# Attention and a gated MoE layer on one core: the portions in which the values' matmuls are queued

## What is computed

```python
scores = scale * np.matmul(q, k.transpose(0, 1, 3, 2))
psi_rel = np.log1p(np.abs(rel))
psi_i = np.log1p(np.maximum(pos[:, None].astype(np.float32), 1.0))
x = (psi_rel / psi_i)[..., None]
h = np.maximum(x @ w1 + b1, 0.0)
bias = h @ w2
scores = scores + bias.transpose(2, 0, 1)[None, :, :, :]
scores = scores - np.max(scores, axis=-1, keepdims=True)
attn = np.exp(scores)
attn = attn / (np.sum(attn, axis=-1, keepdims=True) + 1e-09)
return np.matmul(attn, v).astype(np.float32)
...
gate = 1.0 / (1.0 + np.exp(-(x @ w_gate)))
val = x @ w_val
return (gate * val @ w_out).astype(np.float32)
```

## Time and profile before

| | before |
|---|---|
| median of 3 runs | 822.9 us (821.3 to 824.1) |
| the profiled execution | 825.04 us |
| its span, first to last instruction | 823.2 us |
| TensorE busy | 782.6 us (95%) |
| VectorE busy | 332.0 us (40%) |
| ScalarE busy | 338.0 us (41%) |
| GpSimd busy | 194.9 us (24%) |
| values' matmuls (L882), share of the chain that ended last | 10% |
| mean granted clock of TensorE | 0.987 |

### The profile page before, as it was taken

One profiled execution on the slowest core, in us unless ns is written; L12 is line 12 of the kernel. 1 busy time (PEld: TensorE's weight loads), 2 busy tenths in 40 slices (PEclk: granted clock), 3 DMA queues, 4 the chain that ended last, 5 costly groups with the idle time before them and its releaser, 6 DMA issues.

```text
span 823.2 us, 13263 instructions
## 1 busy us (share of the span) xinstructions
PE 782.6 (95%) x5008; PEld 627.8 (76%) x5008; DVE 332.0 (40%) x797; ACT 338.0 (41%) x683; POOL 194.9 (24%) x362
## 2 busy tenths in 40 slices
PE   5684999999999999999989999999999999999998
PEld 2232666666666666669978998999899889989996
DVE  5894766666666666633320221123022202211220
ACT  5794666666666666643321221122022212212210
POOL 0000666646545545668400000000000000000000
PEclk9998999999999999999989999999999999999999
DMA  6684233242242233213322000100010010000001
GB/s 157 167 204 129 57 102 84 72 106 62 67 121 60 66 85 84 62 55 98 115 76 77 1 1 14 64 1 1 27 52 1 14 64 1 1 26 14 1 2 38
DMA packets 89152, 49.91 MB, mean 61 GB/s; under 512 B 60928, under 2 KB 80512, under 8 KB 89088
## 3 DMA queue, kind: packets, MB, share of 16 engines
q1 hardware_dynamic: 89088, 49.06, 21.9%
HBM read 28.98 MB, written 9.44 MB: 47 GB/s over the span
## 4 chain that ended last, share of the span: by engine, by line
PE 84%; DMA 5%; DVE 3%; ACT 3%; POOL 2%; SPq 1%; issue 1%; POOLq 0%; DVEq 0%; ACTq 0%
PE f_ps L950 18%; PE g_ps L900 15%; PE u_ps L900 15%; PE v_ps L882 10%; PE so_ps L816 9%; PE ty_ps L829 4%; PE tx_ps L841 3%; PE so_ps L811 2%; DVE feats L656 2%; DMA w_raw<-in_w_gate 2%; DMA x_raw<-in_w_out 2%; PE so_ps L764 2%; POOL w L480 1%; DMA bias<-bias_rows 1%; ACT feats L524 1%
## 5 line engine op out<-in xcount | busy, mean ns | idle before, releaser
L559 ACT ACTIVATE probs<-neg_scores,neg_max 128x576 f32<-128x576 f32 x144 | 110.6, 770 | 93.0 <-DVE neg_max L671 93.0
L900 PE MATMUL g_ps<-x_h,w 128*128 128x384 f32 x576 | 146.6, 335 | 1.2 <-DVE hid L733 1.2
L900 PE MATMUL u_ps<-x_h,w 128*128 128x384 f32 x576 | 146.3, 334 | 0.0
L733 DVE TENSOR_TENSOR hid<-u_ps,sig 128x384 f32<-128x384 f32 x72 | 40.1, 557 | 244.7 <-PE u_ps L900 244.7
L671 DVE CUSTOM_DVE_ANT_0 neg_scores<-so_ps,bias 128x576 f32<-128x576 f32 x144 | 104.0, 756 | 75.8 <-PE so_ps L816 54.6
L463 POOL TENSOR_SCALAR probs<-probs,recip 128x512 f32<-128x512 f32 x128 | 89.0, 695 | 187.6 <-DVE recip L685 187.6
L900 PEld LDWEIGHTS g_ps<-x_h,w 128*128 128x128 f32 x576 | 103.9, 188 | 2.3 <-DVE hid L733 1.6
L900 PEld LDWEIGHTS u_ps<-x_h,w 128*128 128x128 f32 x576 | 103.9, 188 | 0.5 <-issue 0.5
L620 ACT ACTIVATE h_h<-hid 128x384 fp32r<-128x384 f32 x72 | 37.9, 527 | 149.0 <-DVE hid L733 149.0
L900 PE MATMUL g_ps<-x_l,w 128*128 128x384 f32 x288 | 96.3, 334 | 0.0
L900 PE MATMUL u_ps<-x_l,w 128*128 128x384 f32 x288 | 96.2, 334 | 0.0
(11 more groups left out here) (68 smaller groups left out, 989.3 us busy)
## 6 DMA issues: line engine op xcount, KB each, us to landing
bias<-bias_rows SPq DMA_DIRECT2D x64, 144.0 KB
x_raw<-attn_transposed SPq DMA_DIRECT2D x6, 768.0 KB, 4.6
out<-out_sb SPq DMA_DIRECT2D x18, 256.0 KB, 2.0
q_raw<-in_q SPq DMA_DIRECT2D x32, 128.0 KB, 2.6
k_raw<-in_k SPq DMA_DIRECT2D x32, 128.0 KB, 2.5
v_main<-in_v SPq DMA_DIRECT2D x32, 128.0 KB, 2.3
w_raw<-in_w_gate SPq DMA_DIRECT2D x12, 256.0 KB, 2.9
w_raw<-in_w_val SPq DMA_DIRECT2D x12, 256.0 KB, 2.9
```

The source lines that it names most:

```text
L559: nc.scalar.activation(probs[s % RING][:, place, :], neg_scores[s % 2][:, place, :], ACT.Exp, bias=neg_max[:, stat(s, place)], scale=-1.0, ...
L733: nc.vector.tensor_tensor(hid[f % 2][:, :], u_ps[f % 3][:, 0:CH], sig[f % 2][:, :], ALU.mult).then_inc(gated, 1)
L900: last = nc.tensor.matmul(bank[f % 3][:, 0:CH], w[:, f, part, i, t, :], x[:, t, :], start=m == 0, stop=m == len(terms) - 1)
```

## The change

The same tiles are multiplied in other portions. Group 0: tiles 0 to 2 at m=4 and tiles 3 and 4 at m=0 of the next pair, where it was 0 and 1 at m=4, 2 and 3 at m=0, and 4 at m=1. Group 1: all five tiles at m=2 of the next pair, where it was 0 to 2 at m=2 and 3 and 4 at m=3. The call ahead of the transposes of m=1 goes.

```diff
-        VALUE_SLOTS = {4: (0, 0, (0, 1)), 0: (1, 0, (2, 3)), 1: (1, 0, (4,)), 2: (1, 1, (0, 1, 2)), 3: (1, 1, (3, 4))}
+        VALUE_SLOTS = {4: (0, 0, (0, 1, 2)), 0: (1, 0, (3, 4)), 2: (1, 1, (0, 1, 2, 3, 4))}
...
             for s in range(STEPS + DRAIN):
                 pair, m = divmod(s, SPP)
-                back, group, tiles = VALUE_SLOTS[m]
-                of, c = pair - back, s - LAG
+                back, group, tiles = VALUE_SLOTS.get(m, (0, 0, ()))
+                of, c = pair - back if tiles else -1, s - LAG
                 if s < STEPS:
                     scores(s)
-                if m == 1 and of >= 0:
-                    values(of, group, tiles)
...
-                if m != 1 and of >= 0:
+                if of >= 0:
                     values(of, group, tiles)
```

## The result

The changed kernel takes 827.87 us in the median of 6 runs (826.54 to 830.18), the kernel before, with it on the same chip, 822.46 (821.3 to 824.1). The ratio is 1.0071, with a 95% interval of 1.0056 to 1.0086: slower by 5.4 us, where 5.2 was forecast. The profiled execution took 830.2 us (span 828.4).

The account below looks back on a forecast made before the run. TensorE, busy throughout steady attention, was taken as the bound. Fourteen pairs at +0.34 us (+4.8), first pair +0.43, last +0.92 and the end -0.9 gave +5.2 us: 828.1 from the 822.9 median, range 825.4 to 831.4.

Parts of the forecast that it names:

- m=1: Attention step of each steady pair losing its portion of one tile: -0.58 us, to 2.85, just above the 2.79 floor.
- the tails' copy: ScalarE copy that the transposes of m=1 wait for: ready at 1.14 against 1.17 us, priced at nothing, bounds 0 to +0.15 a pair.
- m=2: Attention step of each steady pair getting two more tiles of 320 columns in one portion: +1.06 us, to 5.13.
- m=3: Attention step losing two tiles and a portion: -0.74 us instead of -1.23, since the next scores wait for shifts until 2.79.
- m=4: Attention step getting one tile of 256 columns, +0.43, and waiting for ScalarE's move, +0.17: together +0.60 us, to 3.77.
- ScalarE's move: Move of m=1, which frees the bank for the transposes of m=4: late there, +0.17 us a pair, bounds 0 and +0.17.
- the rival with gains: "Only the portions count": decides if m=3's second shift ends before 2.30 us after the scores' start; 817.5 us, 5%.
- The last pair: Last attention pair, its m=1 already at the floor: taking the tile out saves nothing, so this pair costs +0.92 us.
- the end: After the attention loop: values done ahead of the gate part, weight load 0.9 us earlier, bounds -0.6 and -2.3.
- Only the portions count: Rival, whole attention: m=3's shifts done before TensorE returns, two portion starts saved a pair, 5.1 us plus 0.3; 817.5 us; 5%.
- Gain and loss balance: Rival: the move of m=1 doesn't delay m=4 (-2.4) and attention's end returns 2.3 us (-1.4): 824.3 us, no measurable change; 12%.
- More is late: Rival: m=1's transposes miss the tails' copy, with an echo in m=2, +4.2 us: 832.3; or a chunk meets transfers worse; 10%.

Follow-up runs that it names:

- earlier move: Against the changed kernel, ScalarE's move of m=1 stands between the two exponentials of m=3 instead of behind them; 825.27 us, 1.0043 to the kernel before.
- group 0's part: Against the kernel before, only the first 256 queries' values regrouped: tiles 0 to 2 at m=4, 3 and 4 at m=0; 818.9 us, ratio 0.9963.
- group 1's part: Against the kernel before, only the other 320 queries' values regrouped into one portion at m=2; 828.63 us, ratio 1.0083.
- group 0 at once: Against the kernel before, the first 256 queries' five tiles in one portion at m=0, the other 320 queries unchanged; 818.83 us, ratio 0.9959.
- three: Changed kernel with row step's scores in other banks, ScalarE's move between m=3's exponentials, values copy ahead of them; 819.39 us, 0.9967 to the kernel before.

## Why the prediction was right

**The bound.** TensorE had no idle microsecond in the steady pairs, so every term was to be paid in full, and was.

**m=1** was to give 0.58: it gave 0.58, without a wait. The margin of 0.03 before the tails' copy held: the copy ends at 208.00 (207.68+0.32), 0.99 us after the scores' start at 207.01, and the transposes started at 208.19, 1.18 after it. The upper bound of 0.15 was not needed.

**m=2** was to cost 1.06 and cost 1.08: five tiles of 320 took 2.84 us. Over 14 pairs this makes the 0.3 us by which the forecast was short.

**m=3** was to give back 0.74 instead of 1.23, by the row of the first pair: 2.79 was forecast and measured. A bare step in the trace of the kernel before was the whole evidence. The 2.30 for TensorE's own account was a little high: with the shift's wait lifted the step took 2.21. No term of the sum hangs on it.

**m=4** was to cost 0.60: 3.77 was forecast and measured. The 0.17 of ScalarE's move went away alone in the kernel with the earlier move.

**The tie of the two waits was not seen.** The prediction has the shift's wait (0.49 of m=3) and the move's 0.17 as two prices that add up. As a sum this is right. As a cause it is half right: with the shift's wait lifted nothing is gained, since ScalarE's move ends 4.30 us after the start of m=3 in any case, and the transposes that need it start at 4.44. What m=3 gives back then, m=4 takes: 0.58 us either way. The prediction's sentence that only the shift's end decides the rival with gains (before 2.30) was therefore too little: the move, VectorE's move and the copy of the values behind them would have had to be early too. With a bare m=3, the shift's wait and ScalarE's move both lifted, the pair was 17.76, no shorter than before the change.

**The last pair and the ends.** The last pair's m=1 stayed at 2.79, as forecast. For the end, the last scores, the last store and the load of piece 14 in the changed kernel (it answers to the earlier trace rows):

```profile
362.26 1.24 PE L811 MATMUL so_ps<-qk 128*128 128x288 f32 x4 [0.41 <-DVE neg_max L671]
...
376.65 0.34 SPq L366 DMA_DIRECT2D attn_transposed<-x_half  x1
377.03 0.43 SPq L350 DMA_DIRECT2D w_raw<-in_w_gate  x1
```

The load came 14.77 us after the last scores instead of 15.20, although m=4 has become 0.60 longer in between: 1.03 us earlier, where 0.9 was forecast. The prediction's sign for it (0.9 us earlier against the last scores) was worded wrongly: against them it is 0.43, since the 0.60 of m=4, which the sum counts by itself, lies behind them. Of the 1.03, 0.2 was lost again in the loads and splits on the way to the outputs (49.56 us from that load to the outputs, 49.36 before).

**The rivals.** "Only the portions count" came to pass in group 0's part, where TensorE never waits in the steady pairs; there two portions instead of three gave 0.16 us a pair. The Trainium skill (TensorEngine Tiling (Array Packing), Key Properties) states that changing the tiling mode drains TensorE. The trace agrees in direction: a portion less saved 0.16 us a pair. That the drain is what a start costs, no run here shows. In group 1's part one portion less has the same gain on TensorE's own account, and the waits behind it cost four times that (0.51+0.16 = 0.67 us a pair). "Gain and loss balance" had the end of attention give 2.3; it gave 1.0. "More is late" did not occur.

## What to carry to other kernels

When an engine is the bound and its queue mixes two kinds of work, the second kind may be cover for a round trip through the other engines; before taking it out of a step, look for a step that already runs bare, at the start or the end of the loop, and read its length. A saving of 0.16 us per portion is worth taking where the step stays longer than its round trip (here 2.79 us with two shifts; with one shift a step of 2.19 us had no listed wait). And before lifting a wait, ask which one is ready next: here four stood one behind the other (the shift, VectorE's move, ScalarE's move, ScalarE's copy), and the first one lifted alone was worth nothing.

## What the runs showed of the hardware

Executions of one kernel lie up to 4.6 us apart (the kernel before, 820.28 to 824.83 in one series), and the faster ones tend to have the higher mean granted clock (0.992 against 0.988). In the profiles three places differ that no experiment touches. The first is the start of attention: the first pair's scores of m=1 come between 78.63 and 80.71 us, and why is left open here. The other two go with the granted clock, both behind a stretch in which TensorE idles. One is m=2 of the first pair, behind a wait of 7.7 to 9.3 us that falls in the bias table's transfers: with the same queue it took from 2.78 to 3.63 us in these profiles. The other is the first chunk's outputs, behind a wait of 2.4 to 3.0 us for the output weights. They are 108 instructions in every kernel; the chain of waits gives them, before and in group 0's part,

```profile
420.32 27.53 PE f_ps L950 x108
```

```profile
416.20 24.74 PE f_ps L948 x108
```

and the same 108 take 24.52 us in later chunks. In the kernel before the granted clock was 0.50 from 422 to 426 us:

```profile
422.00:426.00 4.00, 4.00 (x10) 3.03 (x10) 0.52 (x1) 0.85 (x1) 0.00 (x0) 0.50 0.49 172
```

In group 0's part it was 1.00 in all of the first 8 us of its outputs. The length of the idle time does not tell which it will be: 2.58 us came ahead of outputs of 26.38 us in the changed kernel, 2.59 ahead of 27.62 in "group 0 at once", and 2.80 ahead of 24.76 in "three". So what two profiles say of a change of 5 us has to be read without these places.
